# Even chunks' inner products in 64 columns, the old state added on VectorE, the first set scaled on VectorE, and ScalarE's order at the attention's end: one float32 kernel of recurrence and two expert layers

## The reference, cut to what matters

```python
for t in range(S):
    y[:, :, t] = np.einsum('bhd,bhde->bhe', rt, state)
    Sa = np.einsum('bhde,bhe->bhd', state, at)
    state_decay = state * wt[:, :, None, :] - np.einsum('bhd,bhe->bhde', Sa, bt)
    state = state_decay + np.einsum('bhd,bhe->bhde', vt, kt)
...
x = _moe_ref(x=x, **moe_kwargs)        # argmax expert, relu MLP 320-1024-320, softmax gate, sigmoid gate
return _moe2_ref(x=x, **moe2_kwargs)   # the same with a capacity per expert
```

## Time and profile before

| | us |
|---|---|
| median of 3 runs | 1190.72 |
| lowest and highest | 1183.19, 1195.39 |
| the profiled execution's own time | 1190.92 |
| its span, first to last instruction | 1189.2 |
| TensorE busy | 1066.2 (90%) |
| VectorE, ScalarE, GpSimd busy | 572.4, 421.2, 329.7 |

### The profile page before, as it was taken

How to read it: one execution, slowest core, us unless ns; L and a number is a source line. 1 busy time by engine, 2 the same in 40 slices (tenths; PEclk the granted TensorE clock), 3 DMA queues, 4 the chain that set the end, 5 groups by cost and what they waited for, 6 DMA issues and landing times.

```text
span 1189.2 us, 36969 instructions
## 1 busy us (share of the span) xinstructions
PE 1066.2 (90%) x16070; PEld 910.4 (77%) x16070; DVE 572.4 (48%) x864; ACT 421.2 (35%) x575; POOL 329.7 (28%) x279
## 2 busy tenths in 40 slices
PE   2489999899989899889999999997599999988997
PEld 1378888788878898758888888886378888866885
DVE  8555557856557552255677777768611111110111
ACT  0144444554444454314333333331033333323331
POOL 7343445434455310010222222222022222211220
PEclk7678899999999898989999999999799999988999
DMA  5244444454444432340333142331113133333000
GB/s 118 63 108 89 110 88 106 123 121 99 102 89 113 112 64 65 130 134 12 116 122 118 56 129 85 118 114 53 49 34 121 35 120 116 122 116 109 23 12 1
DMA packets 181906, 107.37 MB, mean 90 GB/s; under 512 B 136120, under 2 KB 164800, under 8 KB 181620
## 3 DMA queue, kind: packets, MB, share of 16 engines
q1 hardware_dynamic: 171600, 85.00, 27.5%
q0 software_dynamic: 6016, 16.05, 4.4%
q10 hardware_dynamic: 4132, 3.96, 1.0%
HBM read 87.51 MB, written 22.09 MB: 92 GB/s over the span
## 4 chain that ended last, share of the span: by engine, by line
PE 66%; SPq 16%; DMA 6%; DVE 4%; issue 4%; ACT 2%; POOL 1%; ACTq 0%; POOLq 0%; DVEq 0%
PE pair L1251 22%; PE pair L1232 19%; PE pair L1239 6%; SPq L423 5%; SPq L474 3%; SPq L455 3%; DMA t_dram<-T_rows 2%; PE pair L1219 2%; SPq L436 2%; PE pair L1101 2%; SPq L443 2%; PE bank L1114 2%; PE pair L1050 1%; SPq L483 1%; PE pair L1133 1%
## 5 line engine op out<-in xcount | busy, mean ns | idle before, releaser
L1251 PE MATMUL pair<-abk_own,H_nat 128*128 x992 | 277.8, 433 | 2.0 <-DVE S_nat L1537 1.7
L1232 PEld LDWEIGHTS pair<-H_nat,rvm 128*128 128x128 f32 x1984 | 237.5, 197 | 23.9 <-issue 12.5
L1232 PE MATMUL pair<-H_nat,rvm 128*128 128x128 f32 x1984 | 239.2, 281 | 12.7 <-issue 10.3
L1251 PEld LDWEIGHTS pair<-abk_own,H_nat 128*128 128x128 f32 x992 | 184.0, 190 | 71.8 <-issue 3.2
L722 ACT ACTIVATE rvm<-ring_own 128x2560 f32 x62 | 145.0, 2339 | 102.6 <-issue 80.4
L876 ACT ACTIVATE H_nat<-pair 128x512 f32<-128x512 f32 x62 | 37.0, 597 | 323.6 <-PE pair L1239 323.6
L1537 DVE TENSOR_SCALAR S_nat<-pair,gate_all 128x320 f32<-128x320 f32 x62 | 34.1, 551 | 206.2 <-PE pair L1251 206.2
L1530 DVE TENSOR_SCALAR H_nat<-pair 128x512 f32<-128x512 f32 x62 | 42.5, 686 | 167.3 <-PE pair L1239 152.0
L635 POOL TENSOR_SCALAR_AFFINE_SELECT AG<-AG 64x512 f32<-64x512 f32 x48 | 62.8, 1308 | 142.1 <-ACT AG L722 139.7
L703 POOL DMA_INDIRECT out<-S_nat,token_all x31 | 31.5, 1016 | 246.6 <-DVE S_nat L1537 238.6
L703 POOL DMA_INDIRECT between<-S_nat,token_all x31 | 33.9, 1094 | 233.8 <-DVE S_nat L1548 225.7
(11 more groups left out here) (142 smaller groups left out, 1448.2 us busy)
## 6 DMA issues: line engine op xcount, KB each, us to landing
abk_own<-w SPq DMA_DIRECT2D x16, 1280.0 KB, 8.7
ring_own<-w SPq DMA_DIRECT2D x16, 512.0 KB, 3.6
ring_own<-w SPq DMA_DIRECT2D x32, 256.0 KB, 4.5
t_dram<-T_rows SPq DMA_DIRECT2D x12, 384.0 KB, 3.6
ring_own<-w SPq DMA_DIRECT2D x32, 128.0 KB, 5.1
w_in<-wT SPq DMA_DIRECT2D x48, 80.0 KB
abk_own<-aT SPq DMA_DIRECT2D x24, 160.0 KB
abk_own<-bT SPq DMA_DIRECT2D x48, 80.0 KB
```

Source lines behind the costliest of these rows:

```text
L1232: mm(to, w1_now[:, par, k * F + m * P:k * F + m * P + P], xT[:, (0, 2 - m // 4)[k], :], start=(m % 4 == 0 and k == 0), stop=False, skip_gr ...
L1251: last = mm(bank[5][:, 0:DM], hidT[par][:, k, :], ring2[:, bass.ds(place, 1), k, :].rearrange("p a d -> p (a d)"), start=(k == 0), stop=(k ...
```

## The change

1. `inner` of an even chunk runs twice as many matmuls, each with 64 columns of `UV_in` (U or v) in place of 128; the odd chunk's stay.
2. `state` loses the identity matmuls and their waits; each of its matmuls now starts and stops its own sum. `state_out` adds the old state on VectorE into a new tile `Z_sum` (two instructions), then scales from `Z_sum` (four instructions, as before, but not from PSUM any longer).
3. VectorE scales all of set 0 (`scale_set_0`); GpSimd scales from set 1 on, and clears `rvm` and `ZV`, which VectorE did.
4. `x_out` copies the logits first. In the last chunk `x_out(10)` comes before `u_out` and `ut_out`.
5. `WARM` is 9 in the first layer, 11 in the second.

```diff
-WARM = 11
+WARM = (9, 11)
@@ gpsimd
-            nc.gpsimd.memset(UV_even, 0.0).then_inc(cleared, 1)
+            for t in (UV_even, rvm[:, :], ZV[:, :]):
+                nc.gpsimd.memset(t, 0.0).then_inc(cleared, 1)
...
-                    if gram_set == 0:
-                        scale_first(0)
...
+                    if gram_set:
+                        scale_a(2 * gram_set + 1)
+                        pool.wait_ge(bk_landed[gram_set % 2], 128 * (gram_set // 2 + 1))
+                        for u in (2 * gram_set, 2 * gram_set + 1):
+                            scale_bk(u)
@@ scalar: in x_out the copy to lg_parts now stands before the two to x_stage
+                    if u == NU - 1:
+                        x_out(j - 1)
                     if chain:
                         u_out(u)
                         ut_out(u)
-                    if c == 1 and 0 < j <= NK:
+                    if c == 1 and 0 < j <= NK and u != NU - 1:
                         x_out(j - 1)
@@ tensor, state
-                pe.wait_ge(st_done, 2 * states_upto(u - 1))
-                pe.wait_ge(z_kept, 2 * states_upto(u - 1))
-                for o in range(2):
-                    mm(bank[7][head_rows(o), 0:H * D], ident[:, SIDE[o]:SIDE[o] + D],
-                       Z_diag[:, diag_of(u), :, SIDE[o]:SIDE[o] + D], start=True, stop=False, skip_group_check=True)
+                pe.wait_ge(st_added, 2 * states_upto(u - 1))
                 pe.wait_ge(u_copied, 2 * (u + 1))
...
-                                      ZV[:, u % 4, o, b, a, :], start=False, stop=True, skip_group_check=True)
+                                      ZV[:, u % 4, o, b, a, :], start=True, stop=True)
@@ tensor, inner
+                        for role in range(2 * (c == 0)):
+                            for o in range(2):
+                                q = half_rows(o)
+                                last = mm(pair[2][half_rows(o ^ role), o, at:at + C],
+                                          UV_in[k % 2][q, b, a, c, role ^ o, :],
+                                          r_in[k % 2][q, b, a, rt], start=True, stop=True)
+                        for o in range(2 * (c == 1)):
@@ tensor, routing
-                fill(WARM)
+                fill(WARM[s])
@@ vector
             def clear_rest():
-                for t in (rvm, ZV):
-                    v.memset(t[:, :], 0.0).then_inc(cleared, 1)
...
+            def scale_set_0():
+                dve.wait_ge(f_scanned, 1)
+                dve.wait_ge(ag_cleared, 1)
+                dve.wait_ge(a_landed, 32)
+                for u in range(CC):
+                    for o in range(2):
+                        q = head_rows(o)
+                        v.tensor_tensor(
+                            AG[q, u, o].rearrange("p b a t -> p (b a) t"),
+                            a_in[q, :, :, u * C:(u + 1) * C].rearrange("p b a t -> p (b a) t"),
+                            fruns(0)[q, u::CC, 0:C], ALU.mult).then_inc(a_scaled, 1)
+                dve.wait_ge(bk_landed[0], 128)
+                for u in range(CC):
...
+                    v.tensor_tensor(both, both, ends.unsqueeze(2).to_broadcast([P, 2 * NPAIR, 2, C]), ALU.mult
+                                    ).then_inc(bk_scaled, 1)
@@ vector, state_out
                 dve.wait_ge(st_ready, states_upto(u))
+                dve.wait_ge(z_cleared, 1)
+                dve.wait_ge(z_kept, 2 * states_upto(u - 1))
+                for o in range(2):
+                    q = head_rows(o)
+                    v.tensor_tensor(Z_sum[q], view(7, 2 * NPAIR, D)[q],
+                                    Z_diag[q, diag_of(u), :, SIDE[o]:SIDE[o] + D], ALU.add).then_inc(st_added, 1)
                 dve.wait_ge(end_kept, k + 1)
+                dve.wait_ge(st_added, 2 * states_upto(u))
                 for o in range(2):
                     q = head_rows(o)
                     v.tensor_tensor(
-                        ZV[q, to % 4, o].rearrange("p b a d -> p (b a) d"), view(7, 2 * NPAIR, D)[q],
+                        ZV[q, to % 4, o].rearrange("p b a d -> p (b a) d"), Z_sum[q],
                         end_decay[q, k, c::CC].unsqueeze(2).to_broadcast([D, 2 * NPAIR, D]), ALU.mult
                         ).then_inc(st_done, 1)
...
-                        Z_diag[q, diag_of(to), :, SIDE[o]:SIDE[o] + D], view(7, 2 * NPAIR, D)[q],
+                        Z_diag[q, diag_of(to), :, SIDE[o]:SIDE[o] + D], Z_sum[q],
...
                 if j == SLOTS[0]:
+                    scale_set_0()
                     clear_rest()
```

More of the change, by code:

```diff
@@ L201, in recurrence_and_experts @@
         Q_sb = sb("Q_sb", [P, CC, H, HALF])
+        Z_sum = sb("Z_sum", [P, 2 * NPAIR, D])
         R_sb = sb("R_sb", [P, 2, NPAIR, D])
@@ L327, in recurrence_and_experts @@
         z_kept = sem("z_kept")
+        st_added = sem("st_added")
         z_cleared = sem("z_cleared")
@@ L662, in _ @@
                         pool.wait_ge(r_ready, 2 * gram_set - 3)
-                    scale_a(2 * gram_set + 1)
-                    pool.wait_ge(bk_landed[gram_set % 2], 128 * (gram_set // 2 + 1))
-                    for u in (2 * gram_set, 2 * gram_set + 1):
-                        scale_bk(u)
+                    if gram_set:
[3 more added lines that the diff above has]
+                            scale_bk(u)
                 if nats:
@@ L797, in x_out @@
                     act.wait_ge(x_written[k % 2], 32 * (k // 2))
-                t, s = set_of(k)
-                for b in range(2):
-                    copy(x_stage[:, k % 2, b, :].rearrange("p (a o d) -> p a o d", a=NPAIR, o=2),
-                         pair[2][:, b, :].rearrange("p (a o d) -> p a o d", a=NPAIR, o=2)[:, :, :, 0:D], x_copied)
                 if k >= 2:
@@ L805, in x_out @@
                      pair[2][:, :, :].rearrange("p b (a t) -> p b a t", t=P)[:, :, :, D:D + 2 * E], x_copied)
+                for b in range(2):
+                    copy(x_stage[:, k % 2, b, :].rearrange("p (a o d) -> p a o d", a=NPAIR, o=2),
+                         pair[2][:, b, :].rearrange("p (a o d) -> p a o d", a=NPAIR, o=2)[:, :, :, 0:D], x_copied)
             def write_x(k):
@@ L1307, in decays @@
                                      0.0, ALU.mult, ALU.add).then_inc(f_scanned, 1)
+            def scale_set_0():
[11 more added lines that the diff above has]
+                for u in range(CC):
+                    both = bk_in[0].rearrange("p b a c r t -> p (b a) c r t")[:, :, u]
+                    ends = E_run[:, 0, 2:].rearrange("p (n t) -> p n t", t=C + 1)[:, u::CC, 0:C]
+                    v.tensor_tensor(both, both, ends.unsqueeze(2).to_broadcast([P, 2 * NPAIR, 2, C]), ALU.mult
+                                    ).then_inc(bk_scaled, 1)
             def solve_first(k):
@@ L1369, in state_out @@
                     v.tensor_tensor(
-                        ZV[q, to % 4, o].rearrange("p b a d -> p (b a) d"), view(7, 2 * NPAIR, D)[q],
+                        ZV[q, to % 4, o].rearrange("p b a d -> p (b a) d"), Z_sum[q],
                         end_decay[q, k, c::CC].unsqueeze(2).to_broadcast([D, 2 * NPAIR, D]), ALU.mult
                         ).then_inc(st_done, 1)
-                dve.wait_ge(z_cleared, 1)
                 for o in range(2):
```

## The result

Slower: a median of 1235.35 us over 4 runs of the changed kernel (1228.47 to 1241.56), against 1191.13 over 4 of the kernel before; the ratio is 1.0378, interval 1.03 to 1.0456. The profiled execution took 1241.56 us, its span is 1239.0. (Medians are over all executions; in every comparison here the ratio pairs a kernel's runs with those of the kernel before on the same chip, round by round, and leaves out executions of either that fell in a slower state, so it can lie 0.01 from the quotient of two medians.)

What follows compares the result with a forecast made beforehand. TensorE's own chain and the loop through VectorE, GpSimd and SyncE were taken as about equally long. Terms -3.2 - 3.3 + 7.5 + 15 + 3 = +19 on 1190.9 gave 1210 us; range 1181 to 1238, likeliest case alone 1200 to 1222.

Steps and rivals of the forecast that it cites:

- turns: Rival, chance 0.15: GpSimd instructions run between VectorE's state multiplications, about 3.5 to 4 us a slot, 1233 us.
- The scaling in the even chunk: VectorE's four state multiplications from SBUF meet GpSimd's scaling, one engine standing for the other: +1.5 us a slot, +15.
- The additions in the odd chunk: Additions ahead of VectorE's mask before `corner` delay it: +0.75 us in each of ten slots, +7.5 in all.
- The identity matmuls: Removed ahead of `state`; TensorE waits about 1.0 us for ScalarE's copy of U instead of 0.34: gain 0.
- The even `inner`: 64 small matmuls save at most 0.95 us a chunk; only about 0.2 remains, as `right_side` needs the new state.
- The start: VectorE scales the first set while GpSimd clears, so the first solve comes earlier: -3.2 us, bounds -1 and -4.5.
- The end: Last chunk's `inner` waits less, logits come sooner, a shorter fill lets sorting start earlier: -3.3 us, bounds -0.5 and -3.8.
- The clock: More standing still lets TensorE's half-speed share in the loop grow by a fifth: +3 us, bounds 0 and +15.

Runs made afterwards that it cites:

- the clears waiting: The changed kernel, but GpSimd waits for VectorE's scan of set 0 before it clears `rvm` and `ZV`: median 1226.23 us, ratio 1.0419.
- the sum in PSUM: The changed kernel with its additions, but the sum written back over PSUM bank 7, so no multiplication has two SBUF operands: median 1186.08 us, ratio 1.0.
- half the fill: The changed kernel with GpSimd's clears after VectorE's scan and 8 dead matmuls of 96 columns between even `inner` and `right_side`: median 1223.95 us, ratio 1.031.
- no additions: The changed kernel with `state` and `state_out` of before (identity matmuls back, no `Z_sum`): median 1183.34 us, ratio 1.0031.
- the no-additions kernel with the clears waiting: The changed kernel with `state` and `state_out` of before, and GpSimd's clears after VectorE's scan: median 1184.41 us, ratio 0.9969.
- GpSimd behind the state: The changed kernel, but in slots 0 to 9 GpSimd starts its scaling only when the even chunk's kept state is written: median 1309.57 us, ratio 1.1.
- the additions alone: The kernel before with only the new `state` and `state_out` (`Z_sum` in SBUF): median 1234.07 us, ratio 1.0475.

## Why the prediction was wrong

The sign was right, slower, and so was the place; the size was not: +19 forecast, +44 measured. The mechanism is that of the rival *turns*, to which I gave 0.15. That its time (1233) is so near is in part luck: it charged 38 us for turns where the loop shows 33, 7.5 for the odd additions where `corner`'s waits rose by 3.6, and 3 for a clock that shows no cost in this loop.

- **The step that failed is "The scaling in the even chunk: +1.5 us a slot".** It took VectorE to get its four multiplications in a row once `scale_a` was over. The runs show turns: the `ZV` pair takes 4.17 us beside two `scale_bk`, each multiplication ends with one of them, and the trace of the whole kernel has a mean of 1262 ns in place of 479. What the meeting costs is the difference between the kernel with the clears waiting (period 39.86) and the one with the sum in PSUM (36.85): 3.0 us a slot, 33 in all, where I had put 15. (At the same 61 us at 1.2 GHz, the kernel with half the fill against the sum in PSUM, it is 2.85 a slot, 31 in all.) A part of it I had at nothing: the odd chunks, whose multiplications meet `scale_a`, hold 9 of the 34 us that VectorE lost. The row that should have decided was before my eyes, 6.33 us for two `scale_bk` around one scan: there too the scan had its turn between the two, and nobody got two instructions in a row. Taken singly, `scale_bk` runs 229.20 to 231.38, the scan ends at 233.56, and the second `scale_bk`, on record from 231.46, ends at 235.54, 2.0 behind the scan. At the start of the kernel before, two of VectorE's products end at 37.56 and 39.81, with two `scale_bk` that end at 37.54 and 39.80. I read it as a price for the two engines together and not as an order. The Trainium skill ("SBUF — State Buffer", section "Who interferes with whom") says that the other engine fully blocks for the whole instruction; the trace agrees, and adds what follows when both have a queue: they alternate.
- **Its consequence was under-read too.** I put the delay on GpSimd's `scale_bk` and so on `grams_b`. It fell on `ZV` first: 30 us of wait before `right_side`, none of any size for `scale_bk`. Each turn that VectorE gives up for 0.5 us of its own work is a `scale_bk` of 2.2 to 2.3 us, so the engine with the short instructions pays (4.17 us for 1.01, against 4.57 for 4.45 on GpSimd).
- **The additions in the odd chunk, +7.5.** In the place where I had put it, too high: `corner`'s waits rose by 3.6 us in the window, and with the sum in PSUM they are 2.6 where 2.1 stood. What the additions of all chunks cost without the meeting stays open. With the sum in PSUM against no additions the period differs by 0.4 us (36.85 and 36.46), 4.3 in all; against the no-additions kernel with the clears waiting (35.70) it is 12.7, but these loops had 61, 51 and 27 us at 1.2 GHz, so the clock may be part of it. The medians (1186.08, 1183.34, 1184.41) put it at a few us, and the ratios (1.0, 1.0031, 0.9969) do not tell them apart.
- **The identity matmuls, 0.** Right: in front of `state` TensorE waits for ScalarE's copy, 1.10 us in the timeline for the 1.0 forecast.
- **The even `inner`, 0.2 of 0.95.** Its duration was right, 64 instructions in 1.16 us (at 248.67, and in the sum-in-PSUM kernel at 228.10). Its saving of 0.95 a chunk with the additions gone is shown neither by the periods nor by the medians.
- **The start, -3.2.** Right in the nine profiled executions with this start in which the copy passed (`T_nat` at 45.6 to 46.4 in place of 48.62, so -2.2 to -3.0), wrong in the profiled execution of the changed kernel itself (51.10, +2.5) and in that of GpSimd behind the state (51.09), because of the shut-out copy, of which I had no term.
- **The end, -3.3.** The steps came as forecast, the sum somewhat less. From the last `join_first` to the sorting the eleven profiled executions with the new end took 56.5 to 66.5 us, with 3 to 24 us of it at 1.2 GHz. At the same 17 us of it, the old end took 64.5 (the kernel before) and 65.2 (the additions alone), the new one 62.1 (clears waiting) and 62.9 (half the fill): about -2.3. In the profiled execution of the changed kernel the clock took it back: 24 us at 1.2 GHz (512 to 533 us above all), 66.5. Its rows, against the earlier trace rows: `inner` waits 0.33 and not 1.37, the fill of 18 ends before VectorE's row numbers, which now set the sorting's start, as the step said.

```profile
547.58 2.00 PE L1106 MATMUL pair<-rvm 64*128 64x64 f32 x32 [0.33 <-ACT rvm L724]
...
560.27 9.48 PE L1144 MATMUL bank<-table_sb 128*128 128x512 f32 x18
...
569.17 3.56 DVE L1533 TENSOR_TENSOR F_run<-table_sb,row_i 128x768 f32<-128x768 f32 x4
...
570.18 5.57 PE L1212 MATMUL bank<-T_T,F_run 128*128 128x62 f32 x48 [0.43 <-DVE F_run L1533]
```

- **The clock, +3.** The time at 1.2 GHz rose from 34 to 99 us, far more than a fifth; but with it at 61 and at 31 the kernel took the same time, so no such term shows in this loop. Where the meeting is absent the longer periods go with more time at 1.2 GHz, and at the attention's end too it goes with a longer stretch.

Summed by the runs: +31 to +33 for the meeting, at most +13 for the additions and some 5 back at start and end make +26 to +41. The profiled execution of the changed kernel lost some 9 more, 5 to the stalled copy and 4 to the slow stretch at the attention's end; how many of its other runs did is not known, since they have no trace. So what lifts the median to +44 is open.

## What to carry to other kernels

Before an elementwise operation of VectorE is given a second SBUF operand, look at what GpSimd does in those microseconds; if both have several instructions queued, price it as one GpSimd instruction for each of VectorE's, as long as GpSimd's queue lasts, and not as one wait for the whole set. With one operand left in PSUM (here the sum written over its own bank) the meeting cost nothing. And work taken from TensorE in a loop whose other engines are as long as it can come back as waits for them: read the wait groups for who is late next, not the busy share. Before two single traces are compared, compare their time at 1.2 GHz: the same loop had a period of 36.46 with 51 us of it and 35.70 with 27.

## What was unexpected of the hardware

- A copy of 16 elements a partition, SBUF to SBUF, took 7.76 us on VectorE beside three GpSimd memsets in a row, and 7.45 in the kernel with GpSimd behind the state; in the four other profiled executions with the same order at the start it passed in 0.94 to 1.46 (1.17 in the kernel before). So the same program order gave either, from execution to execution. GpSimd only writes there, and the copy did not get the turns that the multiplications got: the seams between the memsets at 13.9 and 18.2 us passed it by. On record the memsets overlap there by 0.07 us, where two `scale_bk` have 0.07 between them; whether that is the reason is not shown. By the same section of the Trainium skill a copy can use both port pairs and then contends with GpSimd whatever that does; the trace agrees. With GpSimd's long clears behind `f_scanned` they cannot start beside the copy, and in the five profiled executions with that wait it took 0.63 to 1.34.
- Sixty-four instructions in 64x64 tiles spread over four quadrants took 1.16 us, 18 ns each, in `inner` as in `grams_b`. From start to start they stand 15 ns apart on average: 6 to 8 inside a round of the four quadrants, 37 to 39 between most rounds. Where 128x40 tiles gave way to such a group at the full clock (L1127 to L957) the first start came 149 ns after the last one of the group before, where one 64x64 group followed another (L957 to L1064) mostly 38: a change of the tile's shape cost about 0.1 us here.
- TensorE's granted clock fell when its waits grew (99 us at 1.2 GHz in the loop, 61 and 31 with dead matmuls in the waits), with no change in the time: where another engine sets the pace, as in this loop, the clock's mean says who stood still and not what it costs.
